# Who splits the first weights, and when the second weights are rounded, in a TensorE-bound attention and two-layer kernel

## The reference

```python
k_p = k.reshape(B, H, Sp, 8, D).mean(axis=3)          # 8 x 8 heads, S = 576, D = 64
v_p = v.reshape(B, H, Sp, 8, D).mean(axis=3)
attn = softmax(q @ k_p.T / sqrt(D))
x = (attn @ v_p), heads side by side                  # 4608 x 512, float32
h = x @ w_in;  g = h * sigmoid(h);           x = g @ w_out      # layer 1, d_ff = 2048
h = x @ w_in;  g = h * clip(h + 3, 0, 6)/6;  out = g @ w_out    # layer 2
```

## Time and profile before

| | us |
|---|---|
| median of 3 runs (lowest to highest) | 1722.51 (1721.97 to 1722.82) |
| the profiled execution | 1724.1 |
| its span | 1722.3 |

### The profile page before, as it was taken

How to read it: one execution, slowest core, us unless ns; L and a number is a source line. 1 busy time by engine, 2 the same in 40 slices (tenths; PEclk the granted TensorE clock), 3 DMA queues, 4 the chain that set the end, 5 groups by cost and what they waited for, 6 DMA issues and landing times.

```text
span 1722.3 us, 27457 instructions
## 1 busy us (share of the span) xinstructions
PE 1684.0 (98%) x11104; PEld 1511.6 (88%) x11104; DVE 1034.8 (60%) x1567; ACT 725.6 (42%) x1182; POOL 329.8 (19%) x431
## 2 busy tenths in 40 slices
PE   7789999999999999999999999999999999999999
PEld 6769888888989999999999899999998899999998
DVE  5757567556645655555555765555556766666664
ACT  3645555555454533333333444333344533333332
POOL 4176336434303500000005300000006200000000
PEclk9899999999999999999999999999999999999999
DMA  7233334333222322222223311111112322222221
GB/s 190 74 104 105 111 94 112 107 98 112 80 77 86 124 85 74 74 74 74 74 74 123 98 50 50 49 50 50 49 50 98 123 74 74 75 79 80 80 78 52
DMA packets 129838, 145.83 MB, mean 85 GB/s; under 512 B 47536, under 2 KB 74416, under 8 KB 129712
## 3 DMA queue, kind: packets, MB, share of 16 engines
q1 hardware_dynamic: 77888, 127.42, 22.6%
q10 hardware_dynamic: 51824, 16.65, 3.9%
HBM read 96.86 MB, written 47.19 MB: 84 GB/s over the span
## 4 chain that ended last, share of the span: by engine, by line
PE 89%; DVE 5%; ACT 2%; issue 1%; DMA 1%; POOL 1%; ACTq 0%; SPq 0%; DVEq 0%; POOLq 0%
PE zw L597 7%; PE zw L599 7%; PE zw L598 7%; PE acc L671 6%; PE xy L597 5%; PE xy L599 5%; PE xy L598 5%; PE acc L673 5%; PE acc L672 5%; PE acc L678 4%; PE acc L677 4%; PE acc L679 4%; PE att L679 4%; PE att L678 4%; PE att L677 4%; PE att L671 2%
## 5 line engine op out<-in xcount | busy, mean ns | idle before, releaser
L1161 DVE TENSOR_TENSOR g_lo<-g_raw,g_hi 128x1024 fp32r<-128x1024 f32 x144 | 196.7, 1368 | 7.8 <-ACT g_raw L877 7.8
L865 ACT COPY x_sum<-xy 128x256 f32<-128x256 f32 x144 | 52.5, 365 | 308.7 <-PE xy L599 308.5
L1128 DVE TENSOR_TENSOR x_sum<-xy,x_sum 128x256 f32<-128x256 f32 x144 | 60.5, 420 | 196.1 <-ACT x_sum L865 196.1
L597 PE MATMUL xy<-xr_hi,w1r_hi 128*128 128x256 f32 x576 | 167.4, 291 | 7.2 <-DVE xs_lo L1200 5.1
L671 PE MATMUL acc<-g_hi,w_hi 128*128 128x512 f32 x400 | 166.4, 416 | 0.0
L599 PE MATMUL xy<-xr_hi,w1r_lo 128*128 128x256 f32 x576 | 163.5, 284 | 0.0
L598 PE MATMUL xy<-xr_lo,w1r_hi 128*128 128x256 f32 x576 | 163.5, 284 | 0.0
L673 PE MATMUL acc<-g_hi,w_lo 128*128 128x512 f32 x400 | 156.9, 392 | 0.0
L672 PE MATMUL acc<-g_lo,w_hi 128*128 128x512 f32 x400 | 156.6, 392 | 0.0
L517 POOL TENSOR_TENSOR w_sum<-w_raw 128x256 f32<-128x256 f32 x16 | 16.1, 1006 | 727.2 <-DMA w_raw<-in_moe_w_in_dram 727.2
L1152 DVE TENSOR_TENSOR g_raw<-zw,x_sum 128x512 f32<-128x512 f32 x144 | 99.0, 688 | 92.2 <-PE zw L599 92.2
(11 more groups left out here) (184 smaller groups left out, 4842.2 us busy)
## 6 DMA issues: line engine op xcount, KB each, us to landing
partial<-y_stage SPq DMA_DIRECT2D x72, 256.0 KB, 2.0
y_part<-partial SPq DMA_DIRECT2D x18, 1024.0 KB, 5.9
x_raw<-first_layer_t SPq DMA_DIRECT2D x18, 1024.0 KB, 7.7
x_raw<-attended_t SPq DMA_DIRECT2D x10, 1024.0 KB, 8.1
first_layer_t<-y_stage SPq DMA_DIRECT2D x36, 256.0 KB, 2.0
out_dram<-y_stage SPq DMA_DIRECT2D x36, 256.0 KB, 2.0
w_raw<-in_moe_w_in_dram SPq DMA_DIRECT2D x16, 512.0 KB, 4.2
kv_stage<-in_v_dram SPq DMA_DIRECT2D x56, 144.0 KB
```

The lines of the kernel that those rows point to most:

```text
L597: nc.tensor.matmul(dst, s_hi[i], m_hi[i], start=first and i == 0, stop=False, skip_group_check=True)
L1161: nc.vector.tensor_tensor(g_lo[:, p], g_raw[:, p % 2], g_hi[:, p].bitcast(fp32), ALU.subtract)\
```

## The change

VectorE splits all four first-weight tiles; GpSimd's split_w1 and its semaphore go, and the load of tiles 2 and 3 waits for VectorE's splits. The places at which ScalarE rounds the first-weight tiles move from 4, 5, U + 12 and U + 16 to 7, U, U + 14 and U + 20, and VectorE's splits are at U + 1, U + 3, U + 16 and U + 22. The second-weight tiles, rounded before at places 1 to 8, one each, are rounded at 2, 3, U, U + 2, U + 5, U + 7, U + 12 and U + 14. In SP's queue the loads of second-weight tiles 2 and 3 come behind the stores of the last step, and the loads of tiles 4 to 7 behind the earlier result and the x block of the first step.

```diff
-W1_ROUND_AT = [4, 5, U + 12, U + 16]
-W1_SPLIT_AT = [U + 18, U + 21]
+W1_ROUND_AT = [7, U, U + 14, U + 20]
+W1_SPLIT_AT = [U + 1, U + 3, U + 16, U + 22]
+W2_AT = [2, 3, U, U + 2, U + 5, U + 7, U + 12, U + 14]
...
-                        sp.wait_ge(w1_split_pool, w1_pool_splits(ps, p - 2))
+                        sp.wait_ge(w1_split, w1_splits(ps, p - 2))
...
             for s in range(STEPS):
                 ps, blk = divmod(s, NB)
-                if ps and blk == 0:
-                    for f in range(4, NF):
-                        load_w2(ps, f)
                 if ps % 2:
                     load_part(s)
...
+                if ps and blk == 0:
+                    for f in range(4, NF):
+                        load_w2(ps, f)
                 if blk == NB - 1 and ps + 1 < PASSES:
                     load_w1(ps + 1, 2)
                     load_w1(ps + 1, 3)
-                    for f in range(4):
+                    for f in (0, 1):
                         load_w2(ps + 1, f)
                 for j in range(NK):
                     store_y(s, j)
+                if blk == NB - 1 and ps + 1 < PASSES:
+                    for f in (2, 3):
+                        load_w2(ps + 1, f)
...
             for ps in range(1, PASSES):
-                sums(ps, 0)
-                sums(ps, 1)
-                split_w1(ps, 0)
-                split_w1(ps, 1)
-                sums(ps, 2)
-                sums(ps, 3)
+                for p in range(NPAIR):
+                    sums(ps, p)
...
-                    if ps and p < 2:
-                        pe.wait_ge(w1_split_pool, w1_pool_splits(ps, p))
-                    else:
-                        pe.wait_ge(w1_split, w1_splits(ps, p))
+                    pe.wait_ge(w1_split, w1_splits(ps, p))
...
-                    if ps and blk == 0 and 1 <= place <= NF:
-                        round_w2(ps, place - 1)
+                    if ps and blk == 0 and place in W2_AT:
+                        round_w2(ps, W2_AT.index(place))
...
-                        split_w1(ps + 1, 2 + W1_SPLIT_AT.index(place))
+                        split_w1(ps + 1, W1_SPLIT_AT.index(place))
```

More of the change, by code:

```diff
@@ L123 @@
 BEFORE, USED = bank_uses()
-W1_ROUND_AT = [4, 5, U + 12, U + 16]
-W1_SPLIT_AT = [U + 18, U + 21]
+W1_ROUND_AT = [7, U, U + 14, U + 20]
+W1_SPLIT_AT = [U + 1, U + 3, U + 16, U + 22]
+W2_AT = [2, 3, U, U + 2, U + 5, U + 7, U + 12, U + 14]
 def w1_splits(ps, p):
-    return 2 * (p + 1) if ps == 0 else 8 + 4 * (ps - 1) + 2 * (p - 1)
-def w1_pool_splits(ps, p):
-    return 4 * (ps - 1) + 2 * (p + 1)
+    return 2 * (ps * NPAIR + p + 1)
 W2_FIRST_AT = [3, 4, 5, 6, 7, U]
@@ L283, in build @@
         w1_summed = sem("w1_summed")
-        w1_split_pool = sem("w1_split_pool")
         w2_split = sem("w2_split")
@@ L540, in pool_head @@
                 nc.gpsimd.tensor_tensor(dst, src[:, :D], src[:, D:2 * D], ALU.add).then_inc(kv_pooled, 1)
-            def split_w1(ps, p):
-                raw, sums_ = w1_source(ps, p)
-                n = 2 * (ps * NPAIR + p)
-                pool.wait_ge(w1_rounded, n + 1)
-                nc.gpsimd.tensor_tensor(w1r_lo[:, p], raw, w1r_hi[:, p].bitcast(fp32), ALU.subtract).then_inc(w1_split_pool, 1)
-                pool.wait_ge(w1_rounded, n + 2)
-                nc.gpsimd.tensor_tensor(w1s_lo[:, p], sums_, w1s_hi[:, p].bitcast(fp32), ALU.subtract).then_inc(w1_split_pool, 1)
             def split_w2(ps, f):
```

## The result

| | us |
|---|---|
| before, median of the runs beside it (lowest to highest) | 1722.24 (1721.96 to 1722.82) |
| after, median of 4 runs (lowest to highest) | 1742.27 (1739.04 to 1744.71) |
| ratio, 95% interval | 1.0111 (1.0095 to 1.0128) |
| the profiled execution after, and its span | 1744.2, 1742.4 |

A forecast was written before the change was run, and what follows sets the result against it. The prediction took TensorE, busy 98% of the span, as the bound, so only its pauses count. Waits removed -5.4, tile 5 +14.7 and chunk b0 +7.0 give +16.3 on 1722.5, so 1739 us, range 1728 to 1748.

The forecast's parts named there:

- Waits removed: Chunk phases at pass starts and ends: 5.4 of 6.9 us of weight-preparation waits go; 0.75 stays in steps 18 and 27.
- Tile 5: Units of steps 9, 18, 27: second-weight tile 5, rounded behind four x roundings, comes 3.1, 5.8, 5.8 us late; 14.7 together.
- the part without a conflict: Lower bound for second-weight tile 5 from ScalarE's order alone: 3.1, 3.1 and 0.3 us late in steps 18, 27 and 9.
- The price of one conflict: GpSimd's second-weight splits beside VectorE's last split of g and x sums: 1.05 us each, 2.7 us taken in all.
- Not added: Second-weight tiles 2 and 3 also late, tile 3 by 3.2 us in the second layer, but inside tile 5's 5.8 us.
- Chunk b0: Late first-weight splits in steps 8, 17, 26 make TensorE wait in the next step's chunks: 0.9, 2.0, 4.1; 7.0 us.
- The 1.4 us for one of the eight: GpSimd's eight sums of first-weight tiles 2 and 3 in a pass's last step take 1.4 us each beside VectorE.
- The moved loads: SP's queue: two of four second-weight loads no longer precede the stores; part of about 1 us less store wait.
- rival 4: TensorE's clock falls in a new pause, one or two falls, +3.4 to +10 us on the sum: 1742 to 1752; 20%.
- Rivals 1 and 2: First: waits mostly hidden, 1717 to 1720, 4%. Second: GpSimd-VectorE conflicts cost little, 1724 to 1731, 16%.

The follow-up runs named there:

- fill_pauses: Changed kernel plus useless TensorE matmuls in its pauses before chunk b0 and before units of second-weight tiles 2, 3, 5; 1741.0 us, ratio 1.0106.
- short_splits: Changed kernel with GpSimd splitting only 16 of 512 columns of second-weight tiles 2, 3 and 4; 1733.0 us, ratio 1.0062.
- w2_places_back: Changed kernel with second weights rounded at places 1 to 8 again, SP's new queue order kept; 1726.9 us, ratio 1.0024.
- w1_part: Changed kernel with only its first-weight half: second-weight rounding places and loads set back as before; 1736.7 us, ratio 1.0078.
- tile5_early: Changed kernel with second-weight tiles 4 and 5 rounded one and two places earlier, ahead of the x roundings; 1737.1 us, ratio 1.0085.
- stores_first: Changed kernel with all four second-weight loads behind the stores of the last step; 1742.6 us, ratio 1.0111.
- w2_part: Kernel before plus only the second weights' new places, loads of tiles 4 to 7 behind the x block; 1738.8 us, ratio 1.0096.
- late_tile3: Changed kernel with first-weight tile 3 rounded and split at place 0 of the next step; 1738.8 us, ratio 1.0099.
- short_sums: Changed kernel with most of GpSimd's sums of first-weight tiles 2 and 3 left out; 1737.2 us, ratio 1.0085.

## Why the prediction was right, and where its steps were off

The forecast was 1739 us, 16.3 us slower, in a range from 1728 to 1748; measured were 1742.3. By its own steps:

- **Waits removed**, 5.4 us: measured 4.4. Steps 18 and 27 kept 1.1 us each besides b0 and the clock, not 0.75, and steps 9 and 26 0.1 and 0.2.
- **Tile 5**, 5.8 + 5.8 + 3.1 = 14.7 us: measured without the clock 6.3 + 6.3 + 3.5 = 16.1 (the unit phases of fill_pauses), with it 17.4. This step was right in cause and place, and short by 1.4 us in size. Tile 5 was forecast ready at U + 14.6, 17.4 and 17.4 in steps 9, 18 and 27, and TensorE resumed at U + 14.9, 17.7 and 17.7; short_splits confirmed the part without a conflict (U + 15.1 for U + 14.7) and the 2.7 us of conflict (2.6). The price of one conflict, 1.05 us, was right, but all of them fell on the x sums (1.65 to 1.75 us each in place of 0.69); the last splits of g took 2.43 us for two, as without a conflict. "Not added" was right for tiles 2 and 3, too: they waited 2.8 us, within the 6.3.
- **Chunk b0**, 0.9 + 2.0 + 4.1 = 7.0 us: measured 0 + 2.0 + 3.4 = 5.4. In step 17 the sum of VectorE was to end at T + 7.7 and TensorE resumed at T + 7.8. That this fits so well is partly luck: with the load as fast as in fill_pauses there would have been no wait. (The forecast's own figures add up to T + 7.9, too: 961.35 - 957.21 + 4.8 - 1.) In step 8 GpSimd's sums started at U + 9.4 where U + 10.2 was forecast, and the copy for b0 came at T + 4.7, not 5.7: in time. In step 26 they started at U + 12.8, not 13.3, with the copy at T + 8.0, not 8.8. The 1.4 us for one of the eight was right: 1353.06 - 1341.64 = 11.4 for all.
- **The moved loads** were taken as part of 1 us of shorter waits for stores. That is the step whose reason was too weak: given late splits the order in SP's queue is worth 9.8 us (w2_places_back against w1_part). The forecast held because it costed the change whole, in which the two gated by the late split of tile 3 stand behind the stores; with one half of the change alone it would have failed, as the expectation for w1_part did.
- **The clock** (rival 4, 20%) came true, with a size below the one given. It fell three times, behind pauses of about 2 to 2.5 us. Each stretch was 3.4 us long, not 7, and lost at most 1.7 us, not 3.4; one of three was hidden. The 2.9 us that it cost are most of the 3.7 that the forecast lacked; the errors of the other steps are as large, but nearly cancel.

Together: -4.4 + 17.4 + 5.4 + 1.6 (the clock in the chunks of step 18) = 20.0 us, the growth of the span. Against the forecast of 16.3 the waits removed are 1.0 worse, the units 2.7 (1.3 of it the clock), chunk b0 1.6 better, and the clock in the chunks adds 1.6. Rivals 1 and 2 fall: they needed tile 5 by about U + 12, or conflicts that cost little, and the trace shows both otherwise.

What stays open is what makes the runs of the changed kernel differ (1739.0 to 1744.7). The clock can't be the whole of it: the runs of 1744.2 and 1739.0 us both have a mean granted clock of 0.992, and 0.001 of it is 1.7 us. The load of first-weight tile 2 is a candidate, since by the traces it moves b0 of step 18 by up to 2 us, and the clock behind it; but each kernel has the trace of one execution only.

## What to carry to other kernels

Work moved to a "free" place of an in-order queue inherits every wait that stands ahead of it: tile 5 had a place 6.8 us ahead of its use by TensorE's pace (U + 4.8 for U + 11.6) and lay behind four roundings, each of which waits for VectorE. Ask of each moved instruction, DMA issues included, what the last gated instruction ahead of it is, and put what frees the next stage (evacuations, stores) ahead of what is wanted 20 us later. Where two causes stand in series, take away both in one run: either alone may show nothing. In a kernel bound by TensorE count a pause of 2 us with the slow matmuls that may follow it (1.3 to 3.4 us here), and don't expect the sum of two halves of a change. A run that fills a pause with useless work is read against what the pause would have been in that very execution.

## What the runs showed of the hardware

- TensorE's granted clock fell to half behind pauses of 1.9 and 2.5 us in the midst of dense work, and was back after 3.4 or 6.8 us (968.8 and 1002.9 in after; 987.7 in tile5_early). It did not fall behind every such pause, nor behind the same one in every execution. In front of chunk b0 of step 27 the pause was 3.06 to 3.11 us long in five kernels: the clock stayed up behind it in after and short_splits and fell in tile5_early, stores_first and w2_places_back. In front of tile 5 in step 9 it was 2.48 to 2.53 us: the clock stayed up in after, w2_part and late_tile3 and fell in stores_first and short_sums. With the pauses filled by matmuls (fill_pauses) it was up in all three places. The Trainium skill (TensorE: Matmul & The Clock Gate, "HAM oscillation — how this bites in real kernels") describes such falls where matmuls wait for a DMA in every tile; here a single wait of 1.87 us for another engine was followed by one (step 18 of after), and one of 1.89 at the same place in stores_first was not.
- A GpSimd subtraction and a VectorE addition of 512 columns slow each other, from 1.29 to 1.72 us and from 0.69 to between 1.65 and 1.75 us, where they lie beside each other.
- From the issue of the load of first-weight tile 2 (512 KB, a second one right behind it) in step 17 to GpSimd's first sum of it 3.3 to 5.0 us passed, in six kernels with the same code there.
